# Attention kernel: probabilities times V from split fp32r parts, or in plain fp32 in two column halves of the array

## The chip, the cores and the metric

One core of one Trainium2 chip runs the kernel. The metric is the device time of one execution in microseconds (us). The kernel before takes 828.53 us (median of 3 runs, 827.82 to 830.4).

## The reference

Attention over 4 batches of 8 heads, 576 positions and head width 64, then a mixing block on the result. Everything is fp32 in and out. `xt` in the second part is x with its last two axes swapped.

```
q_rot, k_rot = rotate(q), rotate(k)
scores = scale * q_rot @ k_rot^T
attn = exp(scores - max); attn = attn / (sum(attn) + 1e-9)
x = attn @ v                        # heads side by side: (4, 576, 512)
h = xt @ U @ V                      # rank 32, over the positions
u = x + h^T
out = u + relu(u @ w_ch1) @ w_ch2   # 512 -> 2048 -> 512
```

## The kernel before, in words

The program has two phases with no overlap but a few early loads. Phase A (`_phase_a`) makes the attention and u. Phase B (`_phase_b`) multiplies by the two weight matrices and is not touched.

**Number format.** A matmul of type fp32r (the code's F32R) takes rounded fp32 operands. To get near fp32 precision the kernel splits an fp32 tensor into a high part, rounded to fp32r, and a low part, the rest, and adds the products of the parts. A transpose on TensorE is a matmul of the tile with an identity; these are in plain fp32.

**Slots.** Phase A is one loop over slots n, written out for each engine. A head g has five tiles of query rows, t = 0 to 4 (four of 128 rows and one of 64), so slot n is tile n of head n // 5. There are 160 such slots, 40 for each batch, and then the mixing of the last batch goes on for some more. In slot n each engine has its own order of work, with semaphores between them:

- TensorE (PE): the four score matmuls of tile n (L614); in slots t = 2 and t = 4 one half of the queries of probabilities times V for the head before (`times_v`, L586 to L601); the transposes of the probabilities of tile n-1 (L632, and L627 for the last 64 keys of a head); at most one mixing item.
- VectorE (DVE): row maximum of tile n (L508); adding the halves of a PV result (L522); the low part of the transposed probabilities of tile n-2 (`split_p`, L514); mixing.
- ScalarE (ACT): exp of tile n with its row sum (L424); the copy of the lower half of a PV result (`lower_half`, L440); the high part of the transposed probabilities of tile n-1 (`round_p`, L433); the rounding of q, k (L398) and v (L405); mixing.
- GpSimd (POOL): rotation of q and k of the next pair of heads (L348 to L351), their low parts (L356), the low part of v (`split_v`, L360), and low parts of x (L390).
- SyncE (SP): loads (`load`, L255), the moves that stack high and low parts of q and k (L281), stores.

**Transposed probabilities.** The probabilities of a head are turned in six units: units 0 to 3 are the first 512 keys of query tiles 0 to 3, unit 4 (LAST) is the last 64 queries against all keys, unit 5 (TAIL) the last 64 keys. LAST and TAIL are turned together in slot t = 0 of the next head. Each unit is read twice from PSUM: ACT writes the high part into `pth`, then DVE writes the low part into `ptl`.

**Probabilities times V.** The stationary operand of a matmul holds the high part of v in its columns 0 to 63 and the low part in columns 64 to 127 (`v2`), the moving operand is 288 queries of `pth` or of `ptl`. For each half of the queries (c = 0, 1) there are 5 key tiles times 2 parts = 10 matmuls:

```
products = [(kt, part) for kt in range(NT) for part in (pth, ptl)]
nc.tensor.matmul(work(("pv", g, c), 0, P, CH), v2[:, (g // 2) % 2, kt, g % 2],
                 part[:, g % 2, kt, CH * c:CH * c + CH], ...)
```

The result has 128 rows: 64 from the high part of v and 64 from the low part. ACT copies the lower 64 rows to `low`, DVE adds them to the upper 64 and writes `xt`.

**PSUM.** Four banks hold two sets of scores, so scores(n) wait for exp(n-2). The other four are a ring (RING = 4) of one-bank tenants, in the order in which PE writes them: PV halves, turned units, mixing items (`ring_plan`, L86). `_release` (L187) makes PE wait, before it writes tenant j, for the engine that reads tenant j - RING.

**Mixing.** MIX_AT (L54) lists in which of a batch's 40 slots the mixing items of the batch before run: five "natural" transposes (slots 6 to 16), "low_rank" (21), five "residual" and five "transposed" items (23 to 38). Batch 0 has none beside it.

Of the kernel before, what the change touches and what calls it, by code (L numbers as in the profile page):

```python
# [12 lines left out]
P = 128  # L30
# [11 lines left out]
RING = 4  # L42
# [8 lines left out]
PV_START = {2: 0, 4: 1}  # L51
PV_END = {2: 0, 4: 1}
# [22 lines left out]
SPLIT_Q, SPLIT_K, SPLIT_V = 1, 3, 6  # L75
# [10 lines left out]
def ring_plan():  # L86


    plan = []
    for n in range(B * TILES + MIX_END):  # L90
        b, s = divmod(n, TILES)
        g, t = divmod(n, NT)
        if 1 <= g <= B * H and t in PV_START:
            plan.append(("pv", g - 1, PV_START[t]))
        plan += [("turned", *unit) for unit in units_of(n - LAG)]
        if b >= 1:
            plan += [("mix", b - 1, *item) for item in MIX_AT.get(s, [])]
    return plan, {tenant: j for j, tenant in enumerate(plan)}


def build(nc, qk, v, cos, sin, identity, u4, v4, w, scratch_u, scratch_ut, out):
    plan, at = ring_plan()
    with ExitStack() as both:
# [17 lines left out]
        v_loaded = [sem(f"v_loaded{i}") for i in range(2)]  # L121
# [4 lines left out]
        v_hi = sem("v_hi")  # L126
        lo_split = [sem("q_split"), sem("k_split")]
        v_split = sem("v_split")
# [5 lines left out]
        pt_hi = sem("pt_hi")  # L134
        pt_lo = sem("pt_lo")
        pv_done = sem("pv_done")
        pv_low = sem("pv_low")
        pv_out = sem("pv_out")
# [16 lines left out]
        with ExitStack() as a:  # L155
# [31 lines left out]
def _release(eng, j, plan, e):  # L187
# [15 lines left out]
def _phase_a(nc, e):  # L203
    plan, at, ps, ident = e["plan"], e["at"], e["ps"], e["ident"]
    qk, v = e["qk"], e["v"]
    (cos_t, sin_t, raw, stack, vraw, v2, prob, pth, ptl, low, xt, negmax, sums, inv, xn, xh, xl, hs, uts,
     uraw, uh, ul, vmraw, vs) = (e[x] for x in (
         "cos_t sin_t raw stack vraw v2 prob pth ptl low xt negmax sums inv xn xh xl hs uts "
         "uraw uh ul vmraw vs").split())
    first_k = e["first_k"]  # L210
    (consts_loaded, mix_consts, zeroed, raw_loaded, v_loaded, roped, chain, qk_hi, v_hi, lo_split, v_split,
     stacked, scored, maxed, expd, transposed, pt_hi, pt_lo, pv_done, pv_low, pv_out, sums_eps, sums_inv,
     mixed, x_nat, x_hi, x_lo, h_hi, h_ready, u_ready, ut_ready, u_stored, ut_stored) = (e[x] for x in (
         "consts_loaded mix_consts zeroed raw_loaded v_loaded roped chain qk_hi v_hi lo_split v_split "
         "stacked scored maxed expd transposed pt_hi pt_lo pv_done pv_low pv_out sums_eps sums_inv "
# [8 lines left out]
    def work(tenant, p0, p1, n):  # L224
        at_ = (2 * SCORES + at[tenant] % RING) * BANK
        return ps[p0:p1, at_:at_ + n]

    def turned(g, j):

        bank = work(("turned", g, j), 0, P, BANK)  # L230
        if j == TAIL:
            return bank.rearrange("p (c n) -> p c n", c=1), slice(NT - 1, NT), slice(0, BANK)
        if j == LAST:
            return (bank[:, 0:NT * WT[-1]].rearrange("p (c n) -> p c n", c=NT), slice(0, NT),
                    slice(P * (NT - 1), S))
        return bank.rearrange("p (c n) -> p c n", c=NT - 1), slice(0, NT - 1), slice(P * j, P * j + P)

    def pv_of(n, end):

        g, t = divmod(n, NT)  # L240
        halves = PV_END if end else PV_START
        return (g - 1, halves[t]) if n >= 0 and 1 <= g <= NHEADS and t in halves else None
# [8 lines left out]
    with nc.Block() as block:  # L251

        @block.sync
        def _(sp):
            def load(r):  # L255

                if r >= 2:
                    for j in range(2):
                        sp.wait_ge(stacked[r % 2][j], 96 * (r // 2))
                    sp.wait_ge(v_split, r - 1)  # L260
                sp.dma_start(raw[:, r % 2], qk[r]).then_inc(raw_loaded[r % 2], 16)
                sp.dma_start(vraw[:, r % 2, 0:NT - 1], v[r][:, 0:NT - 1]).then_inc(v_loaded[r % 2], 16)
                sp.dma_start(vraw[0:WT[-1], r % 2, NT - 1], v[r][0:WT[-1], NT - 1]).then_inc(v_loaded[r % 2], 16)
# [30 lines left out]
            sp.wait_ge(zeroed, 2)  # L294
# [34 lines left out]
        def _(pool):  # L329
# [8 lines left out]
            cleared = [vraw[:, 0], vraw[:, 1], prob[:, :, S:SP_], xh[D:P, NT - 1].bitcast(F32),  # L338
# [19 lines left out]
            def split_v(r):  # L358
                pool.wait_ge(v_hi, r + 1)
                nc.gpsimd.tensor_tensor(v2[:, r % 2, :, :, 1], vraw[:, r % 2], v2[:, r % 2, :, :, 0],  # L360
                                        ALU.subtract).then_inc(v_split, 1)

            def prepare(r, s):
# [8 lines left out]
                if s == SPLIT_V + 1:  # L372
                    split_v(r)
# [7 lines left out]
            prepare(0, SPLIT_V + 1)  # L381
# [12 lines left out]
        def _(act):  # L394
# [6 lines left out]
            def split_v(r):  # L401
                act.wait_ge(v_loaded[r % 2], 32 * (r // 2 + 1))
                if r >= 2:
                    act.wait_ge(pv_done, 4 * (r - 1))
                nc.scalar.activation(v2[:, r % 2, :, :, 0], vraw[:, r % 2], ACT.Copy).then_inc(v_hi, 1)  # L405

# [5 lines left out]
            split_v(0)  # L412
# [15 lines left out]
            def round_p(g, j):  # L428
                act.wait_ge(transposed, UNITS * g + j + 1)
                if j == 0 and g >= 2:  # L430
                    act.wait_ge(pv_done, 2 * (g - 1))
                source, keys, queries = turned(g, j)
                nc.scalar.activation(pth[:, g % 2, keys, queries], source, ACT.Copy).then_inc(pt_hi, 1)  # L433

            def lower_half(g, c):

                act.wait_ge(pv_done, 2 * g + c + 1)
                if g:
# [490 lines left out]
```

## Time and profile before

| | us |
|---|---|
| median of 3 runs | 828.53 |
| lowest and highest | 827.82, 830.4 |
| span of the profiled execution, first to last instruction | 826.5 |
| first score matmul | 22.25 |
| last score matmul starts | 356.1 |
| first matmul of phase B | 388.74 |
| PE busy in the span | 747.6 |
| DVE busy | 379.0 |
| ACT busy | 377.8 |
| POOL busy | 259.9 |

The profiled execution's time beside its span isn't given on its own; the median of the runs is 2.0 us more than the span, and that is what lies around it. How to read it: "busy" is the union of the instructions of an engine. A matmul's duration has its way through the array in it, so two neighbours overlap, and what a stream of matmuls costs is read from the distance of their starts. "128*64 128x288" is a stationary operand of 128 rows and 64 columns and a moving one of 288 columns. Bracketed at the end of a row of the timeline stands the engine's idle time before it and who ended it.

### The profile page before, as it was taken

What the parts mean: (1) busy time and instruction counts of PE and PEld (TensorE: products, weight loads), DVE (VectorE), ACT (ScalarE), POOL (GpSimd) and SP (SyncE); (2) the same over time, 40 slices, a digit from 0 to 9 for tenths busy, and PEclk for the clock granted to TensorE, in tenths of its full rate; (3) what the DMA queues carried; (4) which work ended last, traced back from release to release, by engine and by line L of the source; (5) the groups of instructions that cost most, each with busy time, mean ns of one, the idle gap of its engine ahead of it and who ended that gap; (6) DMA issues with size and microseconds to landing.
All of it is one profiled execution on the core that took longest, in us unless ns stands there. A gap on an engine that the chain in (4) does not pass through costs nothing.

```text
span 826.5 us, 12614 instructions
## 1 busy us (share of the span) xinstructions
PE 747.6 (90%) x4816; PEld 664.3 (80%) x4816; DVE 379.0 (46%) x645; ACT 377.8 (46%) x831; POOL 259.9 (31%) x182
## 2 busy tenths in 40 slices
PE   0799989899898989883999999999999999999998
PEld 0688979788777988762988888888878888888886
DVE  2689887879877877775111123111141111321112
ACT  1699988889878987754222311111111112111110
POOL 6677768655865676002433310000000000000000
PEclk9999999999999999997899999999999999999999
DMA  7856655576468743445522103100013000030001
GB/s 238 236 159 184 205 159 159 153 216 196 111 171 228 190 123 84 121 140 167 201 92 77 52 1 104 69 1 1 1 55 118 1 1 1 0 115 1 1 1 58
DMA packets 43419, 86.55 MB, mean 105 GB/s; under 512 B 7584, under 2 KB 16992, under 8 KB 40800
## 3 DMA queue, kind: packets, MB, share of 16 engines
q1 hardware_dynamic: 42928, 84.50, 34.9%
q10 hardware_dynamic: 432, 1.25, 0.4%
q8 instruction: 39, 0.64, 0.3%
q14 instruction: 20, 0.16, 0.1%
HBM read 43.25 MB, written 14.16 MB: 69 GB/s over the span
## 4 chain that ended last, share of the span: by engine, by line
PE 51%; DVE 1%; ACT 0%; issue 0%; DVEq 0%
PE ps L867 26%; PE ps L852 25%; DVE utl L806 1%; DVE res L813 1%; ACT hth L797 0%; ACT wh L776 0%; DVE wl L817 0%; DVE htl L825 0%; DVEq L812 0%
## 5 line engine op out<-in xcount | busy, mean ns | idle before, releaser
L825 DVE SCALAR_TENSOR_TENSOR htl<-ps,hth 128x288 fp32r<-128x288 f32 x128 | 58.5, 458 | 349.0 <-ACT hth L797 349.0
L797 ACT ACTIVATE hth<-ps 128x288 fp32r<-128x288 f32 x128 | 52.6, 412 | 347.7 <-PE ps L852 347.7
L852 PE MATMUL ps<-uth,wh 128*128 128x288 f32 x512 | 152.5, 298 | 11.5 <-DVE utl L806 11.5
L852 PE MATMUL ps<-uth,wl 128*128 128x288 f32 x512 | 152.5, 298 | 0.0
L852 PE MATMUL ps<-utl,wh 128*128 128x288 f32 x512 | 152.3, 297 | 0.0
L614 PE MATMUL ps<-stack 128*128 128x288 f32 (+1 forms) x640 | 124.5, 317 | 22.3 <-DMA stack<-raw 22.3
L508 DVE TENSOR_REDUCE negmax<-ps 128x1 f32<-128x576 f32 (+1 forms) x160 | 120.3, 752 | 52.6 <-PE ps L614 51.3
L424 ACT ACTIVATE prob<-ps,negmax 128x576 f32<-128x576 f32 (+1 forms) x160 | 118.4, 740 | 40.6 <-DVE negmax L508 40.0
L867 PE MATMUL ps<-wh,hth 128*128 128x512 f32 (+1 forms) x320 | 125.2, 391 | 5.0 <-DVE res L813 5.0
L867 PE MATMUL ps<-wh,htl 128*128 128x512 f32 (+1 forms) x320 | 125.2, 391 | 0.0
L867 PE MATMUL ps<-wl,hth 128*128 128x512 f32 (+1 forms) x320 | 125.1, 391 | 0.0
L514 DVE TENSOR_TENSOR ptl<-ps,pth 128x512 fp32r<-128x512 f32 (+1 forms) x192 | 121.6, 647 | 4.0 <-ACT pth L433 2.2
L632 PE MATMUL ps<-ident,prob 128*128 128x128 f32 (+1 forms) x672 | 96.5, 268 | 18.3 <-ACT prob L424 16.4
L852 PEld LDWEIGHTS ps<-uth,wh 128*128 128x128 f32 x512 | 97.4, 190 | 17.8 <-issue 10.0
L614 PEld LDWEIGHTS ps<-stack 128*128 128x128 f32 (+1 forms) x640 | 91.4, 183 | 23.8 <-issue 22.2
L433 ACT ACTIVATE pth<-ps 128x512 fp32r<-128x512 f32 (+1 forms) x192 | 105.7, 570 | 2.0 <-PE ps L632 0.7
L852 PEld LDWEIGHTS ps<-utl,wh 128*128 128x128 f32 x512 | 97.5, 190 | 2.4
L632 PEld LDWEIGHTS ps<-ident,prob 128*128 128x128 f32 (+1 forms) x672 | 72.8, 141 | 32.0 <-ACT prob L424 28.0
L852 PEld LDWEIGHTS ps<-uth,wl 128*128 128x128 f32 x512 | 97.4, 190 | 0.0
L597 PE MATMUL ps<-pth,v 128*128 128x288 f32 x320 | 90.7, 306 | 1.0 <-DVE xt L522 0.5
L597 PE MATMUL ps<-ptl,v 128*128 128x288 f32 x320 | 89.7, 302 | 1.0 <-DVE ptl L514 1.0
L763 POOL TENSOR_TENSOR wl<-tables,wh 128x1024 fp32r<-128x1024 f32 (+1 forms) x16 | 38.0, 2378 | 107.3 <-ACT wh L776 107.3
(63 smaller groups left out, 888.0 us busy)
## 6 DMA issues: line engine op xcount, KB each, us to landing
stack<-raw SPq DMA_DIRECT2D x192, 144.0 KB, 2.6
raw<-in_qk SPq DMA_DIRECT2D x16, 1152.0 KB, 5.5
tables<-in_w SPq DMA_DIRECT2D x16, 512.0 KB, 3.6
raw<-scratch_ut SPq DMA_DIRECT2D x4, 1152.0 KB, 7.6
vraw<-in_v SPq DMA_DIRECT2D x16, 256.0 KB, 5.4
scratch_u<-xn SPq DMA_DIRECT2D x16, 256.0 KB, 3.3
scratch_ut<-uts SPq DMA_DIRECT2D x16, 256.0 KB, 3.4
res<-scratch_u SPq DMA_DIRECT2D x16, 256.0 KB, 3.8
```

The source lines that it names most:

```text
L424: nc.scalar.activation(prob[0:w, n % NP, 0:S].rearrange("p (c n) -> p c n", c=2), scores_of(n, w), ACT.Exp, bias=negmax[0:w, n % NT:n % NT ...
L433: nc.scalar.activation(pth[:, g % 2, keys, queries], source, ACT.Copy).then_inc(pt_hi, 1)
L508: nc.vector.tensor_reduce(negmax[0:w, n % NT:n % NT + 1], scores_of(n, w), AX.XY, ALU.max, negate=True).then_inc(maxed, 1)
L514: nc.vector.tensor_tensor(ptl[:, g % 2, keys, queries], source, pth[:, g % 2, keys, queries], ALU.subtract).then_inc(pt_lo, 1)
L597: mm = nc.tensor.matmul(work(("pv", g, c), 0, P, CH), v2[:, (g // 2) % 2, kt, g % 2], part[:, g % 2, kt, CH * c:CH * c + CH], start=(kt, p ...
L614: mm = nc.tensor.matmul(ps[0:w, at_:at_ + CH], stack[:, r % 2, i, 0, P * t:P * t + w], stack[:, r % 2, i, part, CH * c:CH * c + CH], start ...
L632: mm = nc.tensor.transpose(bank[:, c], prob[0:w, (NT * g + j) % NP, P * c:P * c + P], ident[0:w, 0:w])
L763: nc.gpsimd.tensor_tensor(wl[:, f, parts], stage(f)[:, parts], wh[:, f, parts], ALU.subtract).then_inc(w_lo, 1)
L797: nc.scalar.activation(hth[:, i % 2, CH * c:CH * c + CH], ps[:, up_bank(j):up_bank(j) + CH], ACT.Relu).then_inc(relu_hi, 1)
L825: nc.vector.scalar_tensor_tensor(htl[:, i % 2, CH * c:CH * c + CH], ps[:, up_bank(j):up_bank(j) + CH], 0.0, hth[:, i % 2, CH * c:CH * c + CH],
L852: mm = nc.tensor.matmul(ps[:, up_bank(j):up_bank(j) + CH], l[:, f, 0, P * d:P * d + P], r[:, CH * c:CH * c + CH], start=(d == 0 and q == 0 ...
L867: mm = nc.tensor.matmul(ps[0:w, BANK * t:BANK * t + DM], l[:, i % 2, P * t:P * t + w], r[:, f, 1], start=(f == 0 and q == 0), stop=(f == F ...
```

## The change

The product of probabilities and V is made of plain fp32 operands. The two halves of the queries go to the two column halves of the array: c = 0 uses 64 stationary columns whose result lies in partitions 0 to 63, c = 1 the same 64 columns of v with the result in partitions 64 to 127 of the same PSUM bank. So there are 10 matmuls for a head instead of 20: key tiles 0 to 2 in slot t = 2 and key tiles 3 and 4 in slot t = 4. The transposed probabilities are kept once, in fp32 (`pt`). Units 1 and 4 are copied by ACT, units 0, 2, 3 and 5 by DVE. V is used as it was loaded, from four buffers (`vt`), with no split on ACT and POOL. The result's left half is copied to `xt` by ACT and the right half by DVE, with no addition. The result has a bank of its own and the ring has three banks. SP's loads no longer wait for the clearing on POOL at the start, nor for the split of v; the load of v waits for PV of three pairs before. The TAIL transposes take 64 stationary columns instead of 128. Cut to its core:

```diff
-RING = 4
+RING = 3
-PV_START = {2: 0, 4: 1}
-PV_END = {2: 0, 4: 1}
+PV_AT = {2: (0, 1, 2), 4: (3, 4)}
+PV_LAST = max(PV_AT)
+VB = 4
+ACT_UNITS = (1, 4)
+DVE_UNITS = (0, 2, 3, 5)
...
-            vraw = sb("vraw", [P, 2, NT, 2, D])
-            v2 = sb("v2", [P, 2, NT, 2, 2, D], F32R)
+            vt = sb("vt", [P, VB, NT, 2, D])
-            pth = sb("pth", [P, 2, NT, S], F32R)
-            ptl = sb("ptl", [P, 2, NT, S], F32R)
-            low = sb("low", [D, 2, CH])
+            pt = sb("pt", [P, 2, NT, S])
...
-    if kind == "turned":
-        eng.wait_ge(e["pt_lo"], UNITS * i + rest[0] + 1)
-    elif kind == "pv":
-        eng.wait_ge(e["pv_out"], 2 * i + rest[0] + 1)
+    if kind == "turned" and rest[0] in ACT_UNITS:
+        eng.wait_ge(e["pt_act"], len(ACT_UNITS) * i + ACT_UNITS.index(rest[0]) + 1)
+    elif kind == "turned":
+        eng.wait_ge(e["pt_dve"], len(DVE_UNITS) * i + DVE_UNITS.index(rest[0]) + 1)
...
+    def pv_bank(c):
+        return ps[D * c:D * c + D, 2 * SCORES * BANK:2 * SCORES * BANK + CH]
...
-                    sp.wait_ge(v_split, r - 1)
+                if r >= VB:
+                    sp.wait_ge(pv_done, 2 * (r - VB + 1))
...
-            sp.wait_ge(zeroed, 2)
...
-            def split_v(r):
-                pool.wait_ge(v_hi, r + 1)
-                nc.gpsimd.tensor_tensor(v2[:, r % 2, :, :, 1], vraw[:, r % 2], v2[:, r % 2, :, :, 0],
-                                        ALU.subtract).then_inc(v_split, 1)
...
-                nc.scalar.activation(pth[:, g % 2, keys, queries], source, ACT.Copy).then_inc(pt_hi, 1)
+                nc.scalar.activation(kept, source, ACT.Copy).then_inc(pt_act, 1)
...
+            def keep_left(g):
+                b, h = divmod(g, H)
+                act.wait_ge(pv_done, g + 1)
...
+                nc.scalar.activation(xt[D * (h % 2):D * (h % 2) + D, b % 2, h // 2, 0:CH], pv_bank(0),
+                                     ACT.Copy).then_inc(pv_left, 1)
...
+                source, kept = turned(g, j)
+                nc.vector.tensor_copy(kept, source).then_inc(pt_dve, 1)
...
+                nc.vector.tensor_copy(xt[D * (h % 2):D * (h % 2) + D, b % 2, h // 2, CH:S],
+                                      pv_bank(1)).then_inc(pv_right, 1)
...
+            def times_v(g, t):
+                r, i = divmod(g, 2)
+                if t == min(PV_AT):
+                    pe.wait_ge(v_loaded[r % VB], 32 * (r // VB + 1))
+                    pe.wait_ge(pt_act, len(ACT_UNITS) * (g + 1))
+                    pe.wait_ge(pt_dve, len(DVE_UNITS) * (g + 1))
+                    if g:
+                        pe.wait_ge(pv_left, g)
+                        pe.wait_ge(pv_right, g)
+                for kt in PV_AT[t]:
+                    for c in range(2):
+                        mm = nc.tensor.matmul(pv_bank(c), vt[:, r % VB, kt, i], pt[:, i, kt, CH * c:CH * c + CH],
+                                              start=(kt == 0), stop=(kt == NT - 1))
+                if t == PV_LAST:
+                    mm.then_inc(pv_done, 1)
```

## Rows read from the trace of the kernel before

**Rows 1.** The page's head and first part: span; busy us, share, instructions.

```profile
span 826.5 us, 12614 instructions
PE 747.6 (90%) x4816; PEld 664.3 (80%) x4816; DVE 379.0 (46%) x645; ACT 377.8 (46%) x831; POOL 259.9 (31%) x182
```

**Rows 2.** Stretches: window, length, busy PE, PEld, DVE, ACT, POOL; clock, DMA share.

```profile
74.62:92.26 17.64, 17.02 (x133) 15.74 (x132) 15.66 (x27) 17.07 (x40) 12.72 (x9) 1.00 0.63 179
...
110.30:198.00 87.70, 79.64 (x582) 72.24 (x581) 70.65 (x118) 74.32 (x168) 57.19 (x42) 0.98 0.65 178
```

**Rows 3.** Groups by line and shape: busy us, mean ns; idle before, releaser.

```profile
L514 DVE TENSOR_TENSOR ptl<-ps,pth 128x512 fp32r<-128x512 f32 x160 | 108.8, 680 | 3.8 <-ACT pth L433 2.1
...
L433 ACT ACTIVATE pth<-ps 128x512 fp32r<-128x512 f32 x160 | 95.5, 597 | 2.0 <-PE ps L632 0.7
...
L597 PE MATMUL ps<-ptl,v 128*128 128x288 f32 x320 | 89.7, 302 | 1.0 <-DVE ptl L514 1.0
L632 PE MATMUL ps<-ident,prob 128*128 128x128 f32 x512 | 79.9, 279 | 15.3 <-ACT prob L424 13.7
...
L522 DVE TENSOR_TENSOR xt<-ps,low 64x288 f32<-64x288 f32 x64 | 28.5, 445 | 10.0 <-ACT low L440 9.1
L440 ACT ACTIVATE low<-ps 64x288 f32<-64x288 f32 x64 | 26.1, 408 | 4.6 <-PE ps L597 3.1
...
L514 DVE TENSOR_TENSOR ptl<-ps,pth 128x320 fp32r<-128x320 f32 x32 | 15.3, 480 | 0.2 <-ACT pth L433 0.2
...
L433 ACT ACTIVATE pth<-ps 128x320 fp32r<-128x320 f32 x32 | 13.9, 435 | 0.0
```

**Rows 4.** Timeline of a head of batch 0: start us, us, engine, line, work.

```profile
93.37 0.77 PE L614 MATMUL ps<-stack 128*64 128x288 f32 x4
...
93.98 0.30 PE L597 MATMUL ps<-pth,v 128*128 128x288 f32 x1
...
94.81 0.74 DVE L508 TENSOR_REDUCE negmax<-ps 64x1 f32<-64x576 f32 x1
...
95.31 0.60 PE L632 MATMUL ps<-ident,prob 128*128 128x128 f32 x4
...
95.67 0.78 PE L614 MATMUL ps<-stack 128*128 128x288 f32 x4
...
96.47 0.52 PE L632 MATMUL ps<-ident,prob 64*128 64x64 f32 x5
...
98.13 0.76 DVE L508 TENSOR_REDUCE negmax<-ps 128x1 f32<-128x576 f32 x1
...
98.24 0.66 PE L632 MATMUL ps<-ident,prob 128*128 128x128 f32 x4
...
98.66 0.77 PE L614 MATMUL ps<-stack 128*128 128x288 f32 x4
...
99.27 0.29 PE L597 MATMUL ps<-pth,v 128*128 128x288 f32 x1
```

**Rows 5.** Waits of PE, 22 to 400 us: us in total, times, longest.

```profile
PE ps L632 <- ACT prob L424: 16.4, 27, 2.4
...
PE ps L663 <- DVE hs L559: 4.1, 4, 1.5
PE ps L627 <- DVE xt L522: 2.9, 3, 1.0
PE ps L663 <- DVE ptl L514: 2.4, 3, 0.8
PE ps L663 <- DVE xt L522: 2.3, 3, 0.8
```

**Rows 6.** Timeline: ScalarE in slot 11 of batch 2.

```profile
209.41 0.68 ACT L398 ACTIVATE raw<-raw 128x576 fp32r<-128x576 f32 x1 [2.90 <-POOL raw L351]
```

**Rows 7.** Timeline: SyncE's first load.

```profile
2.08 0.38 SPq L261 DMA_DIRECT2D raw<-in_qk  x1
```

**Rows 8.** Timeline: TensorE after the last score matmul, in the last head's PV.

```profile
361.11 0.40 PE L597 MATMUL ps<-ptl,v 128*128 128x288 f32 x1 [0.84 <-DVE ptl L514]
```

More of the change, by code:

```diff
@@ L120, in build @@
         raw_loaded = [sem(f"raw_loaded{i}") for i in range(2)]
-        v_loaded = [sem(f"v_loaded{i}") for i in range(2)]
+        v_loaded = [sem(f"v_loaded{i}") for i in range(VB)]
         roped = [sem("q_roped"), sem("k_roped")]
@@ L224, in work, with pv_of, pv_ends @@
     def work(tenant, p0, p1, n):
-        at_ = (2 * SCORES + at[tenant] % RING) * BANK
+        at_ = (2 * SCORES + 1 + at[tenant] % RING) * BANK
         return ps[p0:p1, at_:at_ + n]
+    def pv_bank(c):
+        return ps[D * c:D * c + D, 2 * SCORES * BANK:2 * SCORES * BANK + CH]
     def turned(g, j):
-        bank = work(("turned", g, j), 0, P, BANK)
+        bank = work(("turned", g, j), 0, WT[-1] if j == TAIL else P, BANK)
+        i = g % 2
         if j == TAIL:
-            return bank.rearrange("p (c n) -> p c n", c=1), slice(NT - 1, NT), slice(0, BANK)
+            return bank.rearrange("p (c n) -> p c n", c=1), pt[0:WT[-1], i, NT - 1:NT, 0:BANK]
         if j == LAST:
[L234 to L238, printed above, removed]
+            return (bank[:, 0:NT * WT[-1]].rearrange("p (c n) -> p c n", c=NT), pt[:, i, :, P * (NT - 1):S])
+        return bank.rearrange("p (c n) -> p c n", c=NT - 1), pt[:, i, 0:NT - 1, P * j:P * j + P]
+    def pv_of(n):
         g, t = divmod(n, NT)
-        halves = PV_END if end else PV_START
-        return (g - 1, halves[t]) if n >= 0 and 1 <= g <= NHEADS and t in halves else None
+        return g - 1 if n >= 0 and 1 <= g <= NHEADS and t in PV_AT else None
+    def pv_ends(n):
+        return pv_of(n) if n % NT == PV_LAST else None
     def mixes_of(n):
@@ L470, in _ @@
                         mix(*item)
-                for unit in units_of(n - LAG):
-                    round_p(*unit)
+                for g, j in units_of(n - LAG):
+                    if j in ACT_UNITS:
+                        keep_p(g, j)
+                if pv_ends(n) is not None:
+                    keep_left(pv_ends(n))
                 if r + 1 < NPAIRS:
@@ L509, in row_max, with keep_p, keep_right @@
                                         AX.XY, ALU.max, negate=True).then_inc(maxed, 1)
[L511 to L517 removed]
+            def keep_p(g, j):
+                dve.wait_ge(transposed, UNITS * g + j + 1)
+                if j == DVE_UNITS[0] and g >= 2:
+                    dve.wait_ge(pv_done, g - 1)
+                source, kept = turned(g, j)
+                nc.vector.tensor_copy(kept, source).then_inc(pt_dve, 1)
+            def keep_right(g):
                 b, h = divmod(g, H)
[L519 removed]
+                dve.wait_ge(pv_done, g + 1)
                 if h == 0 and b >= 2:
                     dve.wait_ge(mixed, mix_number(b - 2, "natural", NT - 1) + 1)
[L522 to L524 removed]
+                nc.vector.tensor_copy(xt[D * (h % 2):D * (h % 2) + D, b % 2, h // 2, CH:S],
+                                      pv_bank(1)).then_inc(pv_right, 1)
+                if h == H - 1:
                     if b:
@@ L567, in _ @@
                     row_max(n)
-                if pv_of(n - 1, 1):
-                    add_halves(*pv_of(n - 1, 1))
-                for unit in units_of(n - LAG - 1):
-                    split_p(*unit)
+                if pv_ends(n - 1) is not None:
+                    keep_right(pv_ends(n - 1))
+                for g, j in units_of(n - LAG - 1):
+                    if j in DVE_UNITS:
+                        keep_p(g, j)
                 for item in mixes_of(n - 1):
@@ L584, in _ @@
             pe.wait_ge(consts_loaded, 48)
-            def times_v(g, c, second):
-                products = [(kt, part) for kt in range(NT) for part in (pth, ptl)]
-                if not second:
-                    _release(pe, at[("pv", g, c)], plan, e)
-                    pe.wait_ge(v_split, g // 2 + 1)
-                if c == 0:
-                    pe.wait_ge(pt_lo, UNITS * g + (TAIL + 1 if second else -(-CH // P)))
-                mine = products[NT:] if second else products[:NT]
-                for kt, part in mine:
-                    mm = nc.tensor.matmul(work(("pv", g, c), 0, P, CH), v2[:, (g // 2) % 2, kt, g % 2],
-                                          part[:, g % 2, kt, CH * c:CH * c + CH],
-                                          start=(kt, part) == products[0], stop=(kt, part) == products[-1])
-                if second:
+            def times_v(g, t):
[12 more added lines that the diff above has]
+                if t == PV_LAST:
                     mm.then_inc(pv_done, 1)
@@ L674, in _ @@
                     scores(n)
-                for second in (0, 1):
-                    if pv_of(n, second):
-                        times_v(*pv_of(n, second), second)
+                if pv_of(n) is not None:
+                    times_v(pv_of(n), n % NT)
                 for unit in units_of(n - LAG):
```

77 lines of the change are left out of this document (24 added, 53 removed).

## The prediction

> **What bounds the kernel now.** I read the page's head first: 826.5 us span, and PE is busy for 90% of it, twice as long as any other engine [rows 1]. The change touches phase A alone, so a mean over the span says little; I went on to the stretches. In batch 0, where no mixing runs, a pair of heads takes 17.64 us, 8.82 us a head, and PE is busy for 17.02 of them, ACT for 17.07, DVE for 15.66 [rows 2]. The reader is to see three engines close to full at once. With mixing, batch 1 takes 87.70 us with 79.64 of PE [rows 2]: 10.96 us a head, and 1.0 us a head in which PE has nothing.
>
> Then the timeline of one head, by the distance of starts [rows 4]. Ten PV matmuls take 1.33 us (93.98 to 95.31), 0.133 each. Four score matmuls take 0.61 (98.66 to 99.27), the four transposes of a unit 0.36 (95.31 to 95.67). A head has five sets of scores (3.05), 20 PV matmuls (2.66), four such units (1.44), LAST and TAIL (about 0.45 and 0.41): 8.0 us. So some 0.8 of the 8.82 us is waiting, in two places. The first transposes after scores(0) start 2.57 us after those scores (95.67 to 98.24), with 0.61 + 0.45 + 0.41 + 0.61 = 2.08 us of PE work between: 0.5 us idle for maximum and exp. LAST starts 3.10 us after scores(4) (93.37 to 96.47). There the maximum began at 94.81, though the scores had ended at 94.14: DVE was 0.67 us behind. What an idle ACT and DVE can give is such lateness, not their own time; PE's 8.0 us stay unless PV gets cheaper.
>
> **The change, part by part.**
>
> *PV on PE, the term that decides.* Out go 20 x 0.133 = 2.66 us a head. In come 10 matmuls of 288 columns in plain fp32. No row of before shows one. Nearest below are the fp32 transposes: four last 0.60 us [rows 4], one 0.279 [rows 3], so three distances are 0.32 and one is 0.107 us for 128 columns; 288 columns at that rate are 0.24 us. But a transpose has an identity against it. The kernel makes an fp32 number of two fp32r parts, and a full product of such numbers has four partial products: 4 x 0.133 = 0.53 us, the bound above. Two times 0.24, for the two parts of the stationary operand, is 0.48. I take 0.50. If the halves run side by side, a head costs 5 x 0.50 = 2.5 us (bounds 1.2 and 2.7); one after the other 10 x 0.50 = 5.0 us (4.8 to 5.3). Nothing in the trace shows two matmuls side by side: every one of the kernel before writes to partitions from 0 on. I take side by side, because the two have different stationary columns, different PSUM partitions and no wait between them. So -0.16 us a head, 32 heads: **-5.1 us**. The Trainium skill (FP8 and Floating Point Precision, section TensorE Precision Notes) says that true fp32 takes four passes through the array; no row here shows it, and 4 passes at the fp32r distance are the 0.53 above. The Trainium skill (TensorEngine Tiling (Array Packing), section Key Properties) says that tiles of the array work independently and in parallel, which would make it 2.5 and not 5.0 us.
>
> *Copies.* ACT loses per head three 128x512 copies (of five, 0.597 each), one 64x288 copy (0.408) and its split of v, and keeps one 128x512, LAST (0.435) and one 64x288. DVE's five units of 0.680 and one of 0.480 become four copies; the bounds of one are 0.48 and 0.68 us, and I take 0.60, beside ACT's 0.597 for the same shape; two additions (0.445) become one copy [rows 3]. That is some 2.2 us of ACT and 1.9 of DVE a head, all beside PE, and POOL loses the low part of v, which lies beside PE too. Worth: LAST no longer waits. Undelayed it could start 2.57 us after scores(4), and PE has 0.61 + 1.0 + 0.36 + 0.61 = 2.58 us of work there (two key tiles now stand in slot 4). It had 0.61 + 1.33 + 0.36 + 0.61 = 2.91 against 3.10, so -0.19 x 32 = **-6.1 us**. If PE's work in slot 4 is shorter than 1.0, the wait comes back.
>
> *A new wait.* PV of a head now starts in slot 2 only when all six units are copied, TAIL last. DVE takes TAIL after maximum(1), which started at 98.13 and takes 0.76; with 0.5 to 0.6 for the copy TAIL is there at 99.4 to 99.5, and PV would start at 99.27 [rows 4]. Behind this wait in PE's order stand the next transposes, and behind those exp's release. 0.15 us in the heads that have no mixing item in slot 1, about half: **+2.4 us**.
>
> *Ring of three.* PV leaves the ring, so turned units and mixing have three banks for themselves. A mixing item in slot 1 after one in slot 0 waits for TAIL's copy, and a "transposed" item in slot 0 for unit 3's. Before, waits of this kind were 2.9 + 2.4 + 2.3 us in all, with 4.1 for the low-rank chain, 11.7 together [rows 5]. I count half of these as gone with a faster DVE and ACT: **-5 us** (bounds +4 and -10).
>
> *What stays.* In slot 11 of each batch with mixing ACT waits 2.90 us for the rotation of q on POOL [rows 6], and PE behind it; the longest wait of the transposes is 2.4 us [rows 5]. POOL reaches the rotation only after its low part of x, and the change takes nothing out between. The 0.5 us for exp(0) stays as well.
>
> *Start and end.* SP's first load is issued at 2.08 us [rows 7] after clearing that is no longer waited for; -1 us (bounds -1.3 and 0). In the last head PV waited 0.84 us for DVE's low parts [rows 8]: -0.8 us. SP's new wait for PV of three pairs before is long fulfilled in slot 8; if PV were late, the load of k and q behind it would not be, since it is issued ahead. Phase B: nothing.
>
> Sum: -5.1 - 6.1 + 2.4 - 5 - 1 - 0.8 = -15.6 us. Against the span that is 810.9, and with the 2.0 us around it **813 us**, against a median of 828.53.
>
> **Rivals.**
>
> *One after the other (slower).* PE starts the right half only when the left is through, or the column position brings nothing. Its place is slots 2 and 4 of every head, its price 5.0 instead of 2.66 us: +2.34. LAST's wait (0.19) and a part of the stalls of batches with mixing vanish under it: 2.1 us in 8 heads without mixing, 1.9 in 24 with it, 62 us, less 2 for start and end: 828.5 + 60 = **889 us** (883 at 0.48 and 899 at 0.53 a matmul). It decides from the point where a pair takes over 0.5 + 15.6 / 160 = 0.60 us. For it speaks that no row shows two matmuls beside each other and that PE is nearly the bound; against it, only the layout.
>
> *Side by side, but with a stop at each change of layout.* A matmul of 288 columns lasts 0.302 us [rows 3] and the next starts after 0.133: a stop for the array to empty costs up to 0.17 us. Two PV stretches a head, in and out, are four stops: 4 x 0.17 x 32 = 21.8 us, so **835 us**. Against it: the scores with 64 stationary columns start at 93.37 and PV with 128 columns follows 0.61 us later, just as between scores and PV of 128 columns [rows 4]: no stop. The Trainium skill (TensorEngine Tiling (Array Packing), Key Properties) has this rule, that changing the tiling mode drains TensorE; the rows with 64 columns don't bear it out.
>
> *Gain eaten by the rest.* PV costs what it did (2.66) and the ring of three and the wait for TAIL take what the copies give: 828 us.
>
> **How the numbers follow.** Side by side without stops 0.50, one after the other 0.33, stops 0.10, eaten 0.07. The forecast is the first, 813 us, its own range 800 to 830 (lower with PV at 2.2 and all of the 11.7 us gone, upper with the waits not gone). About 0.3%, 2.5 us, is what a measurement of this kernel can tell from no change. Faster is the first case less its upper edge (0.03) plus the lower side of the last two (0.03): 0.50. Slower is the first rival and two thirds of the stops: 0.40. Same is the rest, 0.10. The range has to reach the second sign: 802 to 893 leaves out the lowest tenth of the first case and, of the first rival, the times near its 899: about 0.15 in all.
>
> **What would show it.** PV matmuls in pairs, starts of two neighbours well under 0.25 us apart and a pair each 0.5 us; slot 2 with 1.5 us of PV and slot 4 with 1.0; a head of batch 0 at about 8.6 us; no wait before LAST, 0.5 us before the transposes of tile 0, a little before PV on a DVE copy; ACT and DVE below 80% in phase A. The forecast is wrong if PV starts are evenly 0.5 us apart, if batch 0's heads take 11 us, or if gaps of 0.17 us stand around each PV stretch.

## The result: 839.3 us, 1.2% slower

The changed kernel takes 839.29 us (median of 4 runs, 838.65 to 841.07). Against the kernel before, timed beside it at 829.46 us, the ratio is 1.0124, with a 95% interval of 1.0103 to 1.0144. The forecast was 813 us. The time is near that of the second rival (835 us, stops at each change of layout), which had a chance of 0.10. In the profiled execution the span went from 826.5 to 836.9 us.

The page's head and first part, after:

```profile
span 836.9 us, 12282 instructions
PE 750.8 (90%) x4816; PEld 616.9 (74%) x4816; DVE 341.1 (41%) x549; ACT 292.4 (35%) x655; POOL 235.5 (28%) x166
```

The relief is there: 85 us less on ACT, 38 less on DVE, 24 less on POOL than in [rows 1]. PE has as many matmul records as before (4816), though 320 calls took the place of 640: a plain fp32 matmul runs as two instructions.

Stretches after: a pair of heads of batch 0, the answer to the first of [rows 2], with the same columns.

```profile
74.78:93.71 18.93, 17.37 (x133) 12.95 (x132) 13.24 (x21) 11.89 (x29) 11.13 (x8) 1.00 0.61 173
```

A pair takes 18.93 instead of 17.64 us, with ACT and DVE now far from full and PE with 1.6 us in which it does nothing (0.6 before). The loss isn't spread evenly. From the starts of the first score matmuls of the heads in the two traces, in us:

| | before | after |
|---|---|---|
| first score matmul | 22.25 | 22.84 |
| batch 0 | 73.42 | 80.60 |
| of these, a head from the third on | 8.81 | 9.49 |
| batch 1 | 87.70 | 88.05 |
| batch 2 | 86.98 | 89.45 |
| batch 3, to its last score matmul | 85.71 | 86.36 |

Groups by line and shape after, the answers to [rows 3]:

```profile
L571 PE MATMUL ps<-pt,vt 128*64 128x288 f32 x640 | 92.5, 419 | 3.3 <-issue 3.0 <-DVE pt L487 0.3
L605 PE MATMUL ps<-ident,prob 128*128 128x128 f32 x512 | 83.0, 285 | 23.7 <-DVE pt L487 15.0 <-ACT prob L393 8.7
L487 DVE COPY pt<-ps 128x512 f32<-128x512 f32 x96 | 65.4, 681 | 1.0
...
L487 DVE COPY pt<-ps 64x512 f32<-64x512 f32 x32 | 21.5, 672 | 0.2 <-PE ps L600 0.2
...
L404 ACT ACTIVATE pt<-ps 128x512 f32<-128x512 f32 x32 | 19.1, 597 | 15.2 <-PE ps L605 14.9
...
L494 DVE COPY xt<-ps 64x288 f32<-64x288 f32 x32 | 14.7, 460 | 3.9 <-PE ps L571 2.9
```

L571 is PV now, L605 the transposes, L487 and L404 the copies of the units. A copy on DVE takes 0.681 us, as long as the subtraction did (0.680). The transposes, which waited almost only for ACT's exp (13.7 of 15.3 us), now wait 15.0 us for a copy on DVE.

TensorE's timeline of one head of batch 0, the answer to [rows 4]:

```profile
72.66 0.77 PE L587 MATMUL ps<-stack 128*64 128x288 f32 x4
73.36 1.19 PE L571 MATMUL ps<-pt,vt 128*64 128x288 f32 x8
74.48 0.66 PE L605 MATMUL ps<-ident,prob 128*128 128x128 f32 x4
74.90 0.77 PE L587 MATMUL ps<-stack 128*128 128x288 f32 x4
75.59 0.52 PE L605 MATMUL ps<-ident,prob 64*128 64x64 f32 x5
76.04 0.63 PE L600 MATMUL ps<-ident,prob 128*64 128x128 f32 x4
76.42 0.77 PE L587 MATMUL ps<-stack 128*128 128x288 f32 x4
77.81 0.63 PE L605 MATMUL ps<-ident,prob 128*128 128x128 f32 x4 [0.62 <-DVE pt L487]
78.20 0.76 PE L587 MATMUL ps<-stack 128*128 128x288 f32 x4
79.13 1.68 PE L571 MATMUL ps<-pt,vt 128*64 128x288 f32 x12 [0.17 <-issue]
80.74 0.66 PE L605 MATMUL ps<-ident,prob 128*128 128x128 f32 x4
```

Three things are to be seen by the distance of starts.

1. **PV runs in pairs.** Eight instructions take 1.19 us, twelve 1.68. In the single starts of the stretch of eight they come two at a time, 7 ns apart, and a new pair starts every 0.243 us (in this stretch of twelve the two are 36 ns apart, at the same distance of pairs). PV costs 10 x 0.243 = 2.4 us a head.
2. **There are stops around it.** Scores(4) to PV is 0.70 us where it was 0.61; single starts show 0.224 between the last score matmul and the first of PV, against 0.136 before. After the last pair the transposes start 0.337 us later, and 0.095 of that is more than a pair takes. The second instructions on both sides are late too, by 0.050 and 0.057. That is 0.29 us a stretch, 0.58 a head. In slot 2 of this head the stop before PV lies in the wait for TAIL; the heads of e4, which has no such wait, show it there too (0.220).
3. **Two waits.** Scores(1) to the transposes of tile 0 is 1.39 us where it was 0.91, and it is DVE's copy that ends it. Scores(2) to PV is 0.93 and not 0.70: PV waits for TAIL.

What DVE did around the first of these two waits, from the timeline of a head earlier:

```profile
66.23 0.76 DVE L479 TENSOR_REDUCE negmax<-ps 128x1 f32<-128x576 f32 x1 [0.89 <-PE ps L587]
...
67.02 0.46 DVE L494 COPY xt<-ps 64x288 f32<-64x288 f32 x1
...
67.51 0.69 DVE L487 COPY pt<-ps 128x512 f32<-128x512 f32 x1
...
68.12 0.74 DVE L479 TENSOR_REDUCE negmax<-ps 128x1 f32<-128x576 f32 x1
...
68.35 0.63 PE L605 MATMUL ps<-ident,prob 128*128 128x128 f32 x4 [0.62 <-DVE pt L487]
```

In a ring of three the order of tenants is unit 3, LAST, TAIL, unit 0: the transposes of tile 0 want the bank of unit 3. DVE copies that only after maximum(0) and the copy of the PV result, so the bank is free at 68.20 and the transposes start at 68.35.

### The profile page after: what moved, and what is told of

The parts are those of the page before. It is cut to its first block, busy times and chain, and to the rows that moved or that the text cites. A ratio compares the mean times of both kernels' runs of the same rounds, so it can differ in the third digit from the quotient of the medians.

```text
span 836.9 us, 12282 instructions
## 1 busy us (share of the span) xinstructions
PE 750.8 (90%) x4816; PEld 616.9 (74%) x4816; DVE 341.1 (41%) x549; ACT 292.4 (35%) x655; POOL 235.5 (28%) x166
## 4 chain that ended last, share of the span: by engine, by line
PE 50%; DVE 1%; ACT 0%; issue 0%; DVEq 0%
PE ps L840 26%; PE ps L825 24%; DVE utl L779 1%; DVE res L786 1%; ACT hth L770 0%; ACT wh L749 0%; DVE wl L790 0%; DVE htl L798 0%; DVEq L785 0%
## 5 line engine op out<-in xcount | busy, mean ns | idle before, releaser
L605 PE MATMUL ps<-ident,prob 128*128 128x128 f32 (+1 forms) x672 | 99.6, 273 | 24.9 <-DVE pt L487 15.0
L605 PEld LDWEIGHTS ps<-ident,prob 128*128 128x128 f32 (+1 forms) x672 | 69.6, 142 | 65.1 <-ACT prob L393 39.4
L571 PE MATMUL ps<-pt,vt 128*64 128x288 f32 x640 | 92.5, 419 | 3.3 <-issue 3.0
L487 DVE COPY pt<-ps 128x512 f32<-128x512 f32 (+1 forms) x128 | 86.9, 679 | 1.2 <-PE ps L600 0.2
L340 POOL TENSOR_TENSOR raw<-raw 128x576 f32<-128x576 f32 x31 | 43.8, 1412 | 91.9 <-ACT raw L374 91.9
L840 PEld LDWEIGHTS ps<-wl,hth 128*128 128x128 f32 (+1 forms) x320 | 56.6, 177 | 16.6
```

The costliest lines, as they stand in the source:

```text
L340: nc.gpsimd.tensor_tensor(x, x, xs, ALU.subtract).then_inc(lo_split[which], 1)
L487: nc.vector.tensor_copy(kept, source).then_inc(pt_dve, 1)
L571: mm = nc.tensor.matmul(pv_bank(c), vt[:, r % VB, kt, i], pt[:, i, kt, CH * c:CH * c + CH], start=(kt == 0), stop=(kt == NT - 1))
L605: mm = nc.tensor.transpose(bank[:, c], prob[0:w, (NT * g + j) % NP, P * c:P * c + P], ident[0:w, 0:w])
L840: mm = nc.tensor.matmul(ps[0:w, BANK * t:BANK * t + DM], l[:, i % 2, P * t:P * t + w], r[:, f, 1], start=(f == 0 and q == 0), stop=(f == F ...
```

## The experiments

The theory after the result had three causes: the stops, 0.58 us a head; the ring wait, 2.91 us from scores(0) to the transposes instead of 2.57; TAIL's copy. The main rival was the price of PV itself: that the halves don't really run side by side. Heads of batch 0 are given as the mean from the third on.

**Do the halves run side by side? e1, all left matmuls of a stretch first, then all right ones.**

```diff
-                for kt in PV_AT[t]:
-                    for c in range(2):
+                for c in range(2):
+                    for kt in PV_AT[t]:
```

> Edit: in each PV stretch all matmuls of the left column half come first, then all of the right half, so that neighbours use the same half and nothing else changes. Theory (the two halves run side by side when they alternate): the starts of the PV instructions, 0.11 to 0.12 us apart in the changed kernel, go to about 0.24, a head's PV from 2.4 to about 4.8 us of PE, and the time to 885 to 910 us. Rival (column halves never overlap, a plain fp32 matmul is simply cheap): starts and time stay as in the changed kernel, 839 us within 3.

Measured: 854.17 us (a single run), between both. TensorE's timeline of e1:

```profile
72.18 2.18 PE L571 MATMUL ps<-pt,vt 128*64 128x288 f32 x12 [0.16 <-issue]
...
76.37 1.20 PE L571 MATMUL ps<-pt,vt 128*64 128x288 f32 x8
```

The stretch of eight takes what it took (1.20 against 1.19 us), though four left instructions stand before four right ones; one after the other they would need seven distances of 0.24 and the last one's 0.41, 2.1 us. The stretch of twelve takes 0.50 us more. The trace doesn't name the half of an instruction, but instructions of one half alone start 0.242 us apart (e9 below), and that sorts the single starts of this stretch into two rows: 72.184, 72.449, 72.692, 72.934, 73.177 and 73.419 for the left half, 72.698, 72.992 and then every 0.243 us for the right. The first right instruction starts 6 ns after the third left one, ahead of three queued left ones; in the stretch of eight it starts 13 ns after the first, again ahead of three. So TensorE starts a later matmul of the free half ahead of queued ones of the busy half, and the edit undid only a part of the pairing. The Trainium skill (TensorE: Matmul & The Clock Gate, section Part 3: Packing small matmuls) says that matmuls start and end strictly in program order; these starts can't come about in that order, and the measurement decides. The expectation failed, since it took the queue to be in order.

**The price without pairing: e6.** Each matmul takes all 128 columns.

```diff
-    mm = nc.tensor.matmul(pv_bank(c), vt[:, r % VB, kt, i], pt[...],
-                          start=(kt == 0), stop=(kt == NT - 1))
+    mm = nc.tensor.matmul(ps[:, 2 * SCORES * BANK:2 * SCORES * BANK + CH],
+                          vt[:, r % VB, kt].rearrange("p i d -> p (i d)"), pt[...],
+                          start=(kt == 0 and c == 0), stop=(kt == NT - 1 and c == 1))
```

> Edit: every PV matmul takes 128 stationary columns (v of both heads of the pair), so the left and right queries can't share the array; both are still made, 20 instructions a head, and are summed into one result of 128 rows. It leaves out the separation of the two halves, so the result is a sum of them. Theory (the left and right matmuls of the changed kernel do run side by side; one after the other each instruction costs 0.24 us): starts evenly 0.24 us apart, PV 4.85 instead of 2.40 us a head, less 0.58 us of stops, and part of it in place of waits: 870 to 895 us. Rival (plain fp32 with 64 columns is fast by itself and pairing gives nothing, so 128 columns cost the same): 830 to 845 us.

Measured: 894.95 us, ratio 1.0783 (1.0750 to 1.0816). TensorE's timeline of e6:

```profile
73.12 3.15 PE L571 MATMUL ps<-pt,vt 128*128 128x288 f32 x12 [0.17 <-issue]
...
78.04 2.10 PE L571 MATMUL ps<-pt,vt 128*128 128x288 f32 x8
```

Twelve instructions in 3.15 us are 0.25 apart, in single starts 0.243 but for the first distance of 0.317. Pairing is real and worth some 56 us here, with the stops that it brings already taken off; the first rival (889 us) priced its own case well, but it isn't this kernel.

**What the stops cost: e5, 128 columns, left queries alone.**

```diff
-                    for c in range(2):
-                        mm = nc.tensor.matmul(pv_bank(c), vt[:, r % VB, kt, i], pt[...],
+                    for c in range(1):
+                        mm = nc.tensor.matmul(ps[:, 2 * SCORES * BANK:2 * SCORES * BANK + CH],
+                                              vt[:, r % VB, kt].rearrange("p i d -> p (i d)"), pt[...],
```

> Edit: one matmul per key tile with 128 stationary columns (v of both heads of the pair) and the left 288 queries, in place of two matmuls with 64 columns in the two column halves. It leaves out the right half of the queries: the second half of each head's result is the other head's v times the left queries. The PE time of PV should be the same (10 instructions of about 0.24 us a head against 20 of 0.12), but the array's column layout never changes. Theory (stops of about 0.09 us on entry and 0.16 us on exit of each PV stretch come from the change of column layout): scores(4) to PV goes from 0.70 to 0.61 us, the 0.16 after PV goes, and the time falls by 8 to 16 us. Rival (the stops belong to plain fp32 matmuls or to the waits in PE's queue): gaps stay, time within 3 us of the changed kernel's.

Measured: 830.26 us, ratio 1.0012 (1.0002 to 1.0022), 9.0 us under the changed kernel. TensorE's timeline of e5:

```profile
73.42 0.78 PE L589 MATMUL ps<-stack 128*64 128x288 f32 x4
74.04 1.13 PE L571 MATMUL ps<-pt,vt 128*128 128x288 f32 x4
75.00 0.60 PE L607 MATMUL ps<-ident,prob 128*128 128x128 f32 x4
75.36 0.77 PE L589 MATMUL ps<-stack 128*128 128x288 f32 x4
76.23 0.52 PE L607 MATMUL ps<-ident,prob 64*128 64x64 f32 x5
```

Scores to PV is 0.62 again, PV to the transposes 0.96, four times 0.24: no stop on either side, with the same PV time. Only half of the 0.58 x 32 = 18.6 us comes back. A head of batch 0 gains 0.45 us (9.04 against 9.49), since in slot 2 PV still waits for TAIL, and there is nothing to gain before it, 0.93 us after the scores in both kernels:

```profile
78.67 0.76 PE L589 MATMUL ps<-stack 128*128 128x288 f32 x4
79.61 1.69 PE L571 MATMUL ps<-pt,vt 128*128 128x288 f32 x6 [0.17 <-issue]
```

LAST, with less PE work before it, waits for exp(4) again in every second head of batch 0, 0.87 us after the scores (75.36 to 76.23) where the changed kernel has 0.69. That costs nothing here, because the transposes of tile 0 are held by the ring wait and start 2.93 us after scores(0), against 2.91. The rest is lost elsewhere: the first two heads take 25.5 instead of 23.7 us (slot 6, see e11), and the 24 heads of the batches with mixing gain only 6.2 us together; why so little wasn't tried.

**Who causes the stop: e9, 64 columns, left half alone.** DVE's copy waits for ACT's and reads the same 64 rows.

```diff
-                    for c in range(2):
+                    for c in range(1):
...
-                dve.wait_ge(pv_done, g + 1)
+                dve.wait_ge(pv_left, g + 1)
...
-                                      pv_bank(1)).then_inc(pv_right, 1)
+                                      pv_bank(0)).then_inc(pv_right, 1)
```

> Edit: only the left column half is used, 10 instructions a head with 64 stationary columns at column 0; both engines copy that result, DVE after ACT. It leaves out the right half of the queries. Theory A (the stop belongs to 64-column fp32 matmuls as such): scores(4) to PV stays 0.22 us instead of 0.13 and the 0.337 after the last pair stays near 0.34. Theory B (the array changes its layout only for a matmul that writes partitions 64 to 127): PV follows scores after 0.13 and the transposes follow after 0.24, as with 128 columns. Both: instructions 0.24 us apart, since neighbours use one half, and the same PV time as in the changed kernel; A gives 836 to 842 us, B 828 to 833 us.

Measured: 836.91 us, ratio 1.0095 (1.0074 to 1.0115). TensorE's timeline of e9:

```profile
73.45 0.77 PE L587 MATMUL ps<-stack 128*64 128x288 f32 x4
74.16 1.19 PE L571 MATMUL ps<-pt,vt 128*64 128x288 f32 x4
75.27 0.66 PE L605 MATMUL ps<-ident,prob 128*128 128x128 f32 x4
```

Theory A: half the instructions in the same 1.19 us, and the stops stay (0.71 before, 0.337 in single starts after), with nothing in the right half. So the stop comes with plain fp32 matmuls of 64 stationary columns. The fp32r score matmuls with 64 columns and the fp32 transposes with 64 columns (L600) have none. These rows misled the forecast.

**The ring wait: e2, unit 3 on ACT in place of unit 1.**

```diff
-ACT_UNITS = (1, 4)
-DVE_UNITS = (0, 2, 3, 5)
+ACT_UNITS = (3, 4)
+DVE_UNITS = (0, 1, 2, 5)
```

> Edit: turned units 3 and 4 are copied by ACT (instead of 1 and 4), units 0, 1, 2 and 5 by DVE. Theory (ring wait: the transposes of tile 0 want the bank of unit 3, which DVE copies only after maximum(0) and the copy of the PV result): the wait of the transposes on the DVE copy, 15.0 us in 21 waits, goes, tile 0's transposes come 2.57 instead of 2.91 us after the scores, a head of batch 0 takes about 9.1 instead of 9.46 us, and the time is 7 to 12 us less than the changed kernel's, 827 to 832 us. Rival (the loss is in the stops around PV alone): within 3 us of 839.

Measured: 830.77 us, ratio 1.0027 (1.0014 to 1.0039), 8.5 us under the changed kernel. Waits of TensorE in us in total, times, longest, first in the changed kernel and then in e2:

```profile
PE ps L605 <- DVE pt L487: 15.0, 21, 1.3
```

```profile
PE ps L605 <- ACT prob L393: 16.8, 32, 3.3
```

The wait on DVE's copy is gone, and a head of batch 0 takes 9.12 us instead of 9.49.

**TAIL's copy: e3, TAIL on ACT, unit 3 still on DVE.**

```diff
-ACT_UNITS = (1, 4)
-DVE_UNITS = (0, 2, 3, 5)
+ACT_UNITS = (1, 4, 5)
+DVE_UNITS = (0, 2, 3)
...
-                if g < 2 and j == ACT_UNITS[-1]:
+                if g < 2 and j == LAST:
```

> Edit: only TAIL (unit 5) moves from DVE to ACT; unit 3 stays on DVE. Theory (the two late copies are separate costs): scores(2) to PV falls from 0.93 to 0.70 us in heads without mixing and the ring wait of tile 0's transposes stays at about 2.9 us after the scores; 3 to 7 us less than the changed kernel, 832 to 836 us. Rival (TAIL's lateness hides behind the ring wait): within 2 us of 839.

Measured: 835.58 us, ratio 1.0064 (1.0048 to 1.0080), 3.7 us less than the changed kernel; 9.22 us a head. By the ratios to the kernel before, which was 0.8 us slower beside these runs, it is 0.0060 or 5.0 us.

**Both: e4, units 3, 4 and 5 on ACT.** The same edit with `ACT_UNITS = (3, 4, 5)` and `DVE_UNITS = (0, 1, 2)`.

> Edit: units 3, 4 and 5 are copied by ACT, 0, 1 and 2 by DVE. Theory (ring wait, 0.34 us a head, and PV's wait for the copy of TAIL behind maximum(1), 0.23 us a head, are both due to the place of these copies on DVE): batch 0's heads take about 8.9 us, scores(2) to PV 0.70 instead of 0.93 us, and the time falls by 12 to 20 us, to 819 to 827 us, below the kernel before. Rival (ACT with three units becomes late and exp waits behind its copies): no more than e2's gain, 830 us or more.

Measured: 825.63 us, ratio 0.9958 (0.9945 to 0.9972): faster than the kernel before. TensorE's timeline of e4:

```profile
76.33 0.77 PE L587 MATMUL ps<-stack 128*128 128x288 f32 x4
77.29 0.66 PE L605 MATMUL ps<-ident,prob 128*128 128x128 f32 x4 [0.18 <-ACT prob L393]
77.70 0.77 PE L587 MATMUL ps<-stack 128*128 128x288 f32 x4
78.39 1.68 PE L571 MATMUL ps<-pt,vt 128*64 128x288 f32 x12
```

The transposes of tile 0 follow scores(1) after 0.96 us (1.39 before the edit) and PV follows scores(2) after 0.69 (0.93).

**Without stops, ring wait and TAIL wait: e7, which is e4 with e5's PV.**

> Edit: units 3, 4, 5 on ACT as in e4, and PV with 128 stationary columns and the left queries alone as in e5 (it leaves out the right half of the queries, as e5 does). Theory (stops cost 0.58 us a head, but LAST then waits about 0.15 to 0.2 us more for exp(4), since less PE work covers it): 0.4 us a head less than e4, 12 to 14 us, 811 to 815 us. Rival (what stops take is slack before exp anyway): within 4 us of e4, 822 to 826 us.

Measured: 813.04 us, ratio 0.9794 (0.9778 to 0.9811), 12.6 us under e4, and 8.30 against 8.82 us a head. TensorE's timeline of e7:

```profile
76.19 0.78 PE L589 MATMUL ps<-stack 128*128 128x288 f32 x4
76.82 1.62 PE L571 MATMUL ps<-pt,vt 128*128 128x288 f32 x6
78.27 0.60 PE L607 MATMUL ps<-ident,prob 128*128 128x128 f32 x4
```

Scores(2) to PV is 0.63 us, and six instructions take 1.45. It leaves out half of PV's result and is no kernel to use, but PE's time for PV is that of the changed kernel, so it says what the stops cost once the ring wait and TAIL's no longer hide a part. LAST's wait still does: it starts 0.84 to 0.88 us after the scores, where e4 has 0.70.

**What the relief of ACT and DVE is worth: e8, every unit copied twice on top of e4.**

```diff
+                nc.scalar.activation(other, source, ACT.Copy)
                 nc.scalar.activation(kept, source, ACT.Copy).then_inc(pt_act, 1)
...
+                nc.vector.tensor_copy(other, source)
                 nc.vector.tensor_copy(kept, source).then_inc(pt_dve, 1)
```

> Edit: on top of e4 every copy of a turned unit is made twice by its engine, first to a spare buffer and then to its place, so ACT has six copies of units a head and DVE six, as in the kernel before; nothing else changes. Theory (the relief of ACT and DVE is what the change gains in the heads with mixing, as was forecast with 11 us): the time rises by 8 to 20 us over e4, 834 to 846 us, most of it in batches 1 to 3. Rival (PE and the exp chain bound the kernel, copies lie beside): within 4 us of e4.

Measured: 861.46 us, ratio 1.0387 (1.0365 to 1.0409), 35.8 us over e4 (a head of batch 0 takes 10.03 us). Theory and rival both had it too small. The batches take 9.0, 8.0, 7.7 and 7.8 us more. My reading is that with a ring of three and PV behind all six copies their speed counts for more than I put on it. The kernel before carried the same number of unit copies in 829 us, with a ring of four and a first half of PV that needed only some of the units; how the 36 us split between those two wasn't tried.

**The start: e10, e4 with SP's first load behind the clearing again.**

```diff
+            sp.wait_ge(zeroed, 2)
             load(0)
```

> Edit: e4 (units 3, 4, 5 on ACT), and SP's first load waits for two of POOL's clearings again, as in the kernel before. Theory (the earlier load takes bandwidth from the tables and the identity, which then land last, and the first scores came 0.6 us later): first score matmul at about 22.3 instead of 22.8 us, time 0.3 to 0.8 us under e4's, ratio to the kernel before 0.993 to 0.997. Rival (no effect of the order of loads): first scores at 22.8 us.

Measured: 824.37 us, ratio 0.9949 (0.9933 to 0.9965), which the intervals don't tell from e4. The first score matmul came at 22.55 us (22.77 in e4); e11 below, with the same start, has 21.97, so one trace doesn't give the size. The ten traces of the early load lie between 22.75 and 22.95, the three of the late one (the kernel before, e10, e11) between 21.97 and 22.55. Why the early load didn't help is in the changed kernel's timeline:

```profile
0.74 0.38 SPq L244 DMA_DIRECT2D raw<-in_qk  x1
...
7.55 0.33 SPq L244 DMA_DIRECT2D raw<-in_qk  x1
...
10.29 0.76 DVE L467 TENSOR_TENSOR raw<-raw,tables 128x576 f32<-128x576 f32 x1 [10.29 <-DMA ident<-in_identity]
```

The load of q and k is issued 1.34 us earlier than in [rows 7] and was there by 7.55, when the next one is issued. But now the tables and the identity, which ACT issues from 0.74 to 1.66 us, land last, and DVE begins at 10.29 us (9.76 before, when it waited for q and k).

**A collision that the freed POOL makes: e11.** The first two heads of the changed kernel take 3.1 us more than before (80.60 - 6 x 9.49 = 23.7 against 73.42 - 6 x 8.81 = 20.6), and those of e4 5.0 us more (25.6). In slot 6 DVE splits U and V of the mixing block. Its timeline in e4:

```profile
36.39 1.98 DVE L550 TENSOR_TENSOR ul<-uraw,uh 128x640 fp32r<-128x640 f32 x1 [0.85 <-ACT vs L456]
38.40 3.71 DVE L552 TENSOR_TENSOR vs<-vmraw,vs 32x576 fp32r<-32x576 f32 x2
42.14 0.76 DVE L479 TENSOR_REDUCE negmax<-ps 128x1 f32<-128x576 f32 x1
```

5.7 us for what took 0.81 + 1.53 before; in the changed kernel it is 0.82 + 3.72. POOL runs its rotation of the third pair at that time (three operations of 1.8 to 2.0 us instead of 1.4). Before, it stood waiting for v, for the split that the change took out. e11 puts a wait in its place, on top of e10:

```diff
                 if s == ROPE_Q:
+                    if r == 2:
+                        pool.wait_ge(mix_consts, 53)
```

> Edit: on top of e10, POOL's rotation for the third pair of heads waits until DVE has split U and V of the mixing block. Theory (GpSimd, which no longer waits for the split of v, runs its rotation at the same time as DVE's three SBUF operations in slot 6, and each then takes two to three times as long: 1.72 + 3.72 us against 0.81 + 1.53 in the kernel before; maximum(7), exp and the transposes queue behind): these three fall to about 0.8 + 1.5 us, the 5.3 us wait of the transposes for exp in that slot shrinks to about 2, and the time falls by 2.5 to 3.5 us, to 820.5 to 822.5 us, ratio to the kernel before 0.989 to 0.993. Rival (DVE is slow there for another reason, or the time is made up later): within 0.7 us of e10.

Measured: 820.45 us, ratio 0.9901 (0.9885 to 0.9918), 3.9 us under e10. DVE's timeline in e11:

```profile
35.53 0.83 DVE L553 TENSOR_TENSOR ul<-uraw,uh 128x640 fp32r<-128x640 f32 x1 [1.20 <-ACT vs L459]
36.39 1.54 DVE L555 TENSOR_TENSOR vs<-vmraw,vs 32x576 fp32r<-32x576 f32 x2
```

The operations are as short as before, the longest wait of the transposes for exp in that part fell from 5.1 to 2.2 us, and the first two heads take 20.3 us (25.9 in e10). This is the fastest full version, 1.0% faster than the kernel before and 2.2% faster than the changed one.

## Why the prediction was wrong

- **PV on PE.** Right in mechanism and size: 0.24 us a partial instruction and two of them a matmul, side by side, 2.4 us a head (forecast 2.5; bounds 1.2 and 2.7). e6 shows what the other way would have cost. The four passes that the Trainium skill (FP8 and Floating Point Precision, section TensorE Precision Notes) gives for true fp32 agree with the two instructions of 0.24 us for one matmul if each instruction makes two, which no run shows.
- **"No stop" is the step that failed.** The prediction put the stops at nothing, because the score matmuls with 64 columns have none around them, and took that as proof that no stop follows a change of layout. PV's plain fp32 matmuls with 64 columns do have them. The rule of the Trainium skill (TensorEngine Tiling (Array Packing), section Key Properties), that changing the tiling mode drains TensorE, agrees with the trace after: 0.29 us a stretch, 0.58 a head, 12.6 us of time (e7 against e4). The rival had 0.17 for each of four stops, 0.68 a head, and 21.8 us. That the time came within 5 us of its 835 is luck in part: it had too much for the stops and nothing for the ring wait below.
- **Ring of three: the second step that failed, a term that was missed.** The prediction looked at mixing items and not at the plain case, where unit 0 wants the bank of unit 3 because LAST and TAIL stand between them. e2 gives 8.5 us for it. "+4" was my upper bound for the whole ring.
- **TAIL's copy before PV.** Forecast 0.15 us in half of the heads, 2.4 us; the trace has 0.23 in 13 heads of 32, those of batch 0 and the ones around a change of batch, which would be 3.0 us. Taking it out gives more, 3.7 us alone (e3) and 5.1 us on top of e2 (e4).
- **LAST's wait.** It did shrink, from 0.80 to 0.69 us after the scores (forecast 0.19, measured 0.11), and e5 shows it come back in every second head of batch 0 when less PE work lies before it, as the text said.
- **Copies.** Forecast 0.60 us for DVE's copy of 128x512, measured 0.681, no less than the subtraction. So DVE's own work on units and results fell by 51 us, 1.6 a head (124.1 + 28.5 to 86.9 + 14.7), and not by 1.9. The prediction counted such relief only as lateness that goes; the 36 us of e8 for doubled copies say that in a kernel of this shape it is worth more.
- **The mixing batches.** Forecast -5 us beside what each head gains. In e7 batches 1 to 3 take 243.4 us against 260.4, -17.0; six like heads of batch 0 give 0.51 each, 12.2 for 24 heads, so 4.8 us are left for mixing, and e4, whose heads of batch 0 take what they took before, has 254.7 there, 5.7 less: right in size. The changed kernel doesn't show it that plainly: its batches 1 to 3 lose 3.5 us, where 24 times the 0.68 of a head of batch 0 would be 16.3. POOL's wait in slot 11 stayed, at 2.49 us in batch 2 of the changed kernel [rows 6].
- **Start and end.** Forecast -1 for the start, measured +0.6 us: the tables land last. Forecast -0.8 for the end: from the last score matmul to the first matmul of phase B it is 31.8 us (32.7 before), right. By the code the load of v waits for PV of the pair four before its own, not three.
- **Slot 6.** Not foreseen: POOL, no longer held by v, collides with DVE. DVE's three operations take 2.2 us more, of the 3.1 that the first two heads lose. e11 gives 3.9 us for it, on top of e10, where it is larger.

In a row of steps, e7 to e4 to e2 to the changed kernel, the times are 813.0 + 12.6 (stops) + 5.1 (TAIL) + 8.5 (unit 3), 839.3 us with rounding. It closes because each term is the difference of two runs, so it proves no term by itself. By the ratios to the kernel before, which allow for e7 having run beside a slower one, the three are 13.6, 5.7 and 8.0 us. That e7 stands at the forecast's 813 is in part chance: e7 gained more for a head of batch 0 than was forecast (0.51 against 0.20), and lost to the slot 6 collision (its first two heads take 25.6 us, 20.6 before) and at the start.

## What to carry to other kernels

Before a resource is given a smaller ring, write out its tenants in order and ask for each who frees the bank that many places back, and when in its engine's order, not only for the rare tenants. A row shows that a layout costs nothing only if it makes that layout: an instruction with as many columns but another type proved nothing here. And when work is taken from an engine that had been waiting, look what it now runs beside.

## What the runs showed of the hardware

- A plain fp32 matmul of 288 columns is two instructions 0.24 us apart, whether 64 or 128 stationary columns (e9, e6). Two with 64 columns in different halves run at once, with starts 7 ns apart and a pair every 0.243 us.
- The free half takes later matmuls ahead of queued ones, in both stretches of e1 ahead of three (inferred from the starts): within eight instructions the order of halves made no difference (1.20 against 1.19 us), within twelve it cost 0.50 us (e1).
- A stretch of 64-column plain fp32 matmuls costs 0.29 us in stops on its two sides, also when only one half is used (e9); fp32r matmuls and fp32 transposes with 64 columns don't.
- DVE's copy of 128x512 from PSUM takes 0.681 us against 0.597 on ACT, no less than its subtraction of two operands (0.680).
- DVE operations on SBUF alone beside POOL's took 1.86 us each instead of 0.77 (3.71 and 1.54 for the two).
